# Exponents of an mLSTM's attention-like product taken off TensorE from the fourth chunk on: maxima spread by DMA, masked by GpSimd, applied by ScalarE

## The reference

```python
for t in range(S):
    m_new = np.maximum(f_gate[:, :, t] + m, i_gate[:, :, t])
    f_stab = np.exp(f_gate[:, :, t] + m - m_new)
    i_stab = np.exp(i_gate[:, :, t] - m_new)
    m = m_new
    C = f_stab * C + i_stab * np.einsum('bhd,bhe->bhde', vt, kt)
    n = f_stab * n + i_stab * kt
    h_tilde = np.einsum('bhde,bhe->bhd', C, qt)
    denom = np.maximum(np.abs(np.einsum('bhd,bhd->bh', n, qt)), 1.0)
    y[:, :, t] = sigmoid(o_gate[:, :, t]) * h_tilde / denom
```

## Time and profile before

| | us |
|---|---|
| median of 3 runs (327.9 to 329.29) | 329.14 |
| the profiled execution, whole | 330.02 |
| its span, first to last instruction | 328.3 |
| PE busy / PEld busy | 311.1 / 297.5 |
| DVE busy | 207.6 |
| ACT busy | 151.7 |
| POOL busy | 53.8 |

### The profile page before, as it was taken

One profiled execution on the slowest core, in us unless ns is written; L12 is line 12 of the kernel. 1 busy time (PEld: TensorE's weight loads), 2 busy tenths in 40 slices (PEclk: granted clock), 3 DMA queues, 4 the chain that ended last, 5 costly groups with the idle time before them and its releaser, 6 DMA issues.

```text
span 328.3 us, 5497 instructions
## 1 busy us (share of the span) xinstructions
PE 311.1 (95%) x1952; PEld 297.5 (91%) x1952; DVE 207.6 (63%) x448; ACT 151.7 (46%) x295; POOL 53.8 (16%) x80
## 2 busy tenths in 40 slices
PE   7879978999999999787999999999899999999996
PEld 3879967999899999577999999999899999999996
DVE  7886798767577656744543388886876448657111
ACT  4945565333313332542212367678867166536000
POOL 8712231212021200340211110140000000000000
PEclk9995999999999999999999999999999999999999
DMA  5992221122214215400004202040000100010011
GB/s 147 282 249 70 84 83 37 47 82 84 85 38 145 79 41 195 128 0 2 1 2 137 55 2 60 1 143 18 2 1 20 43 0 2 20 40 2 20 51 51
DMA packets 11374, 20.92 MB, mean 64 GB/s; under 512 B 1908, under 2 KB 5508, under 8 KB 11348
## 3 DMA queue, kind: packets, MB, share of 16 engines
q1 hardware_dynamic: 11348, 20.58, 21.2%
HBM read 18.53 MB, written 1.97 MB: 62 GB/s over the span
## 4 chain that ended last, share of the span: by engine, by line
PE 80%; DVE 9%; ACT 4%; issue 3%; DMA 2%; POOL 1%; SPq 0%; DVEq 0%; ACTq 0%; POOLq 0%
PE ps_v L1096 18%; PE ps_s L1096 11%; PE ps_e L1096 7%; PE ps_in L1096 7%; PE ps_out L1096 6%; PE ps_t L1096 6%; PE ps_s L1165 5%; PE ps_z L1096 5%; PE ps_in L1174 5%; PE ps_out L1184 3%; PE ps_z L1193 2%; DMA wv_raw<-in_w_v 2%; PE ps_e L1142 1%; PE ps_e L1147 1%; DVE pt L826 1%
## 5 line engine op out<-in xcount | busy, mean ns | idle before, releaser
L1165 PEld LDWEIGHTS ps_s<-qkt 128*128 128x128 f32 x192 | 26.0, 200 | 3.0 <-DMA qkt<-in_qk 1.5
L1165 PE MATMUL ps_s<-qkt 128*128 128x128 f32 x192 | 27.1, 287 | 1.3 <-DMA qkt<-in_qk 1.3
L1174 PEld LDWEIGHTS ps_in<-tok,pt 128*128 128x128 f32 x192 | 25.0, 198 | 0.9
L1068 DVE TENSOR_TENSOR kr<-kr 128x384 f32<-128x384 f32 x32 | 17.7, 557 | 12.5 <-ACT kr L755 12.4
L1174 PE MATMUL ps_in<-tok,pt 128*128 128x42 f32 x192 | 24.8, 281 | 0.0
L578 ACT ACTIVATE et<-ps_e 128x512 f32<-128x512 f32 x24 | 14.3, 595 | 20.7 <-PE ps_e L1147 14.5
L727 ACT ACTIVATE gh<-ut 128x384 fp32r<-128x384 f32 x16 | 8.4, 524 | 32.3 <-DVE ut L1034 32.3
L1096 PE MATMUL ps_v<-win,xth 128*128 128x512 f32 x60 | 21.0, 416 | 1.3 <-DVE xtl L907 1.3
L1096 PE MATMUL ps_v<-xth,win 128*128 128x384 f32 x65 | 19.1, 359 | 2.5 <-ACT vr L584 1.4
L826 DVE TENSOR_TENSOR pt<-ps_s,et 128x512 f32<-128x512 f32 x24 | 16.5, 688 | 5.7 <-PE ps_s L1165 4.1
L538 POOL TENSOR_TENSOR gl<-ut,gh 128x384 fp32r<-128x384 f32 x8 | 9.0, 1121 | 59.0 <-ACT gh L727 59.0
(11 more groups left out here) (292 smaller groups left out, 901.7 us busy)
## 6 DMA issues: line engine op xcount, KB each, us to landing
tok<-in_vk SPq DMA_DIRECT2D x12, 328.0 KB, 4.0
qkt<-in_qk SPq DMA_DIRECT2D x24, 160.0 KB
sp_raw<-in_w_sp SPq DMA_DIRECT2D x6, 384.0 KB, 4.6
osig<-in_og SPq DMA_DIRECT2D x2, 960.0 KB, 9.5
out_y<-ob SPq DMA_DIRECT2D x12, 160.0 KB, 1.8
wv_raw<-in_w_v SPq DMA_DIRECT2D x2, 640.0 KB, 5.3
win_raw<-in_w_in SPq DMA_DIRECT2D x4, 256.0 KB, 6.5
wk_raw<-in_w_k SPq DMA_DIRECT2D x2, 512.0 KB, 4.4
```

Of the source, the lines that this page charges most:

```text
L1068: ve.tensor_tensor(kr[n % 4][:, :], kr[n % 4][:, :], kr[n % 4][:, :], ALU.mult).then_inc(sems["kk_done"], 1)
L1165: last = te.matmul(ps_s[j][:, h * CH:(h + 1) * CH], keys[u % NS][:, HH * j + h, :], queries[u % NS][:, h, :], start=True, stop=True)
L1174: last = te.matmul(p_in[:, HH * j + h, :], pt[:, j, h, :], vt[u % 2][:, HH * j + h, :], start=True, stop=True)
```

## The change

- For units 3 to 11 nothing of the exponent is made on TensorE. SP writes the gate maxima `mx` to DRAM (`save_maxima`) and reads them back spread over all 128 partitions into one of two tiles `mb` of 128x1024 (`spread_maxima`).
- GpSimd replaces the entries with s > t by 2^100 (`mask`); it does unit u+1's in slot u, behind inverse_deviation(u−2).
- ScalarE takes eight Exps of 128x128 per unit, one a head: scale −1 on `mb` and the key's a as a bias per partition, from a third group of columns of `gwt`, for which gate_factors copies a once more per chunk.
- `gate_operands` and `gates_lo` (the split of a and −M for TensorE) are left out for chunks 3 to 5, `max_rows` altogether. `mrow` has no batch any more: GpSimd's second memset and head_rows(1, ·) go.
- The batches' gate rows stand closer (GW = 8 instead of 32).
- The u products go to `ps_e` with semaphores of their own (`u_mm`, `u_read`); v products keep `ps_v`.

```diff
-GW = 32
-GR = GW + H
+GW = H
+GR = B * GW
@@ SP
-            def max_rows(u):
...
+            def save_maxima(first, last, signal):
+                sp.wait_ge(sems["gate_m"], last)
+                sp.dma_start(maxima[first:last].rearrange("c r t -> r c t"),
+                             mx[:, first * CH:last * CH].rearrange("r (c t) -> r c t", t=CH)).then_inc(sems[signal], 16)
+
+            def spread_maxima(u):
+                b, c = batch(u), chunk(u)
+                if c < EARLY:
+                    sp.wait_ge(sems["mx_first"], 16)
+                else:
+                    sp.wait_ge(sems["mx_saved"], 16 * (c - EARLY + 1))
+                if u >= EARLY + 2:
+                    sp.wait_ge(sems["exp_done"], 2 * (u - 2) + 2)
+                rows = maxima[c, GW * b:GW * b + H].rearrange("h t -> (h t)")
+                sp.dma_start(mb[u % 2].rearrange("p h t -> p (h t)"),
+                             rows.partition_broadcast(128)).then_inc(sems[f"mx_in{u % 2}"], 16)
...
             for u in range(1, NU):
+                if EARLY <= u + 1 < NC:
+                    save_maxima(u + 1, u + 2, "mx_saved")
+                if u + 1 == NC:
+                    save_maxima(0, EARLY, "mx_first")
                 if EARLY <= u + 1 < NU:
-                    max_rows(u + 1)
+                    spread_maxima(u + 1)
@@ GpSimd
+            def mask(u):
+
+                pool.wait_ge(sems[f"mx_in{u % 2}"], 16 * ((u - EARLY) // 2 + 1))
+                gp.affine_select(out=mb[u % 2][:, :, :], in_=mb[u % 2][:, :, :], compare_op=ALU.is_ge, fill=-NEVER,
+                                 base=0, pattern=[[0, H], [1, CH]],
+                                 channel_multiplier=-1).then_inc(sems["masked"], 1)
...
                 if u >= 2:
                     inverse_deviation(u - 2)
-                if u == 0:
...
-                    head_rows(1, 0)
-                    head_rows(1, 1)
+                if EARLY <= u + 1 < NU:
+                    mask(u + 1)
                 if u in WIN_SLOT:
                     win_lo_of(WIN_SLOT.index(u))
@@ ScalarE
+                sc.activation(gw[64:ER, c, :], am[:, t], ACT.Copy).then_inc(sems["factors"], 1)
 
             def exponentials(u, j):
                 hf = 2 * u + j
-                act.wait_ge(sems["expo_mm"], hf + 1)
                 if hf > 1:
                     act.wait_ge(sems["probs_done"], hf - 1)
-                sc.activation(et[:, j, :, :], ps_e[:, :].rearrange("p (h t) -> p h t", h=HH),
-                              ACT.Exp).then_inc(sems["exp_done"], 1)
+                if u < EARLY:
+                    act.wait_ge(sems["expo_mm"], hf + 1)
+                    last = sc.activation(et[:, j, :, :], ps_e[:, :].rearrange("p (h t) -> p h t", h=HH), ACT.Exp)
+                else:
+                    act.wait_ge(sems["masked"], u - EARLY + 1)
+                    act.wait_ge(sems["gwt_done"], chunk(u) + 1)
+                    for h in range(HH):
+                        x = 64 + GW * batch(u) + HH * j + h
+                        last = sc.activation(et[:, j, h, :], mb[u % 2][:, HH * j + h, :], ACT.Exp,
+                                             bias=gwt[:, chunk(u), x:x + 1], scale=-1.0)
+                last.then_inc(sems["exp_done"], 1)
...
-                if u + 2 < NC:
+                if u + 2 < EARLY:
                     gate_operands(u + 2)
@@ TensorE
             def u_product(g, m):
-                pe.wait_ge(sems["v_read"], V_AT["u", g, m])
-                u_chain(ps_v[:, 0:NB], g, m).then_inc(sems["v_bank_mm"], 1)
+                pe.wait_ge(sems["exp_done"], 2 * EARLY)
+                pe.wait_ge(sems["u_read"], U_AT[g, m])
+                u_chain(ps_e[:, 0:NB], g, m).then_inc(sems["u_mm"], 1)
...
+                if u < EARLY:
+                    exponents(u, 0)
                 if u < NU:
-                    exponents(u, 0)
                     scores(u, 0)
...
+                if u < EARLY:
+                    exponents(u, 1)
                 if u < NU:
-                    exponents(u, 1)
                     scores(u, 1)
```

More of the change, by code:

```diff
@@ L37 @@
 HH = H // 2
-GW = 32
-GR = GW + H
+GW = H
+GR = B * GW
 ER = 64 + GR
+ZR = 64 + D
 NB = 384
@@ L81, in u_tiles @@
     return out
[L84 to L95, removed]
+U_ORDER = [x for slot in range(NU + 2) for x in u_tiles(slot)]
+U_AT = {x: n for n, x in enumerate(U_ORDER)}
 def mlp_groups():
@@ L222, in program @@
     kw = tail("kw", [128, G, 128])
-    nm = tail("nm", [ER, S], F32R)
-    est = tail("est", [ER, NC, CH], F32R)
+    nm = tail("nm", [ER, EARLY * CH], F32R)
+    est = tail("est", [ER, EARLY, CH], F32R)
     gwt = tail("gwt", [128, NC, ER])
@@ L231, in program @@
     zt = [tail(f"zt{n}", [KR, G, 2, DV]) for n in range(2)]
-    zdec = tail("zdec", [ER, G, 2, DV])
+    zdec = tail("zdec", [ZR, G, 2, DV])
+    mb = [at("mb0", [128, H, CH], EP + 12288), tail("mb1", [128, H, CH])]
+    maxima = nc.dram_tensor("maxima", (NC, GR, CH), F32, kind="Internal").ap()
     vr = tail("vr", [128, HF])
@@ L446, in _, with head_rows @@
             gp.memset(rstd[:, 1:2], -0.5)
-            gp.memset(bits(mrow[:, 0, :, :, :]), 0.0).then_inc(sems["rows_zero"], 1)
+            gp.memset(bits(mrow[:, :, :, :]), 0.0).then_inc(sems["rows_zero"], 1)
             pool.wait_ge(sems["rows_zero"], 1)
[L450 to L454, removed]
+            def head_rows(j):
+                for n, r in enumerate((0, 64)):
+                    pool.wait_ge(sems["head_rows_done"], 2 * j + n)
+                    rows = mrow[r:r + H, j, :, :]
                     gp.affine_select(out=rows, in_=bits(rows), compare_op=ALU.not_equal, fill=1.0,
@@ L469, in _ @@
             pool.wait_ge(sems["later_done"], 1)
-            head_rows(0, 1)
+            head_rows(1)
             gp.memset(qkt[:, 2, :], 0.0).then_inc(sems["pad2"], 1)
-            gp.memset(bits(mrow[:, 1, :, :, :]), 0.0).then_inc(sems["rows_one_zero"], 1)
             gp.memset(kw[:, :, :], 0.0).then_inc(sems["kw_zero"], 1)
@@ L1146, in exponents @@
                 pe.wait_ge(sems["later_done"], 1)
-                last = te.matmul(ps_e[:, :].rearrange("p (h t) -> p h t", h=HH), later[:, :],
-                                 ones[:, :].unsqueeze(1).broadcast_to([128, HH, CH]),
-                                 start=False, stop=u >= EARLY)
-                if u < EARLY:
-                    pe.wait_ge(sems["nm_hi_done"], c + 1)
-                    pe.wait_ge(sems["nm_lo_done"], c + 1)
-                    for h in range(HH):
-                        last = te.matmul(ps_e[:, h * CH:(h + 1) * CH],
-                                         mrow[:, b, j, h, 0:1].broadcast_to([ER, CH]),
-                                         nm[:, c * CH:(c + 1) * CH], start=False, stop=h == HH - 1)
+                te.matmul(ps_e[:, :].rearrange("p (h t) -> p h t", h=HH), later[:, :],
+                          ones[:, :].unsqueeze(1).broadcast_to([128, HH, CH]), start=False, stop=False)
+                pe.wait_ge(sems["nm_hi_done"], c + 1)
+                pe.wait_ge(sems["nm_lo_done"], c + 1)
+                for h in range(HH):
+                    last = te.matmul(ps_e[:, h * CH:(h + 1) * CH],
+                                     mrow[:, j, h, 0:1].broadcast_to([ER, CH]),
+                                     nm[:, c * CH:(c + 1) * CH], start=False, stop=h == HH - 1)
                 last.then_inc(sems["expo_mm"], 1)
```

84 lines of the change are left out of this document (35 added, 49 removed).

## The result

The changed kernel takes 325.59 us in the median of 11 runs (323.16 to 327.16), the kernel before 329.14 in 11 (327.77 to 331.88). The ratio is 0.9895, its 95% interval 0.9861 to 0.9929: 3.55 us faster, where 5.6 were forecast. The profiled execution of the changed kernel took 325.59 too, its span is 323.9 against 328.3.

The account below looks back on a forecast made before the run. TensorE was taken to bound slots 5 to 11, then a VectorE-GpSimd-ScalarE loop of 9.58 us per slot. 3.7 by slot 12 plus 1.9 in the tail gave 5.6 us earlier: 324.4 profiled, 323.5 median; range 319.5 to 332.

Parts of the forecast that it names:

- What bounds the kernel: Slots 5 to 11: TensorE is the limit at 10.2 us per slot, VectorE little behind; a new loop becomes the bound.
- The loop: Once per slot through VectorE, GpSimd, ScalarE, VectorE: L895, rstd, mask, Exps, pt to `inter`, handovers; 9.58 us; chance 0.40.
- the step into slot 6: The loop's passage into slot 6, without state_add (−0.66): 8.92 us.
- The spread: The 512 KB spread lands in an estimated 6 us, started some 14 us before mask(u) needs it.
- The bank and the tail: Slots 12 and 13: with its own bank the u product no longer waits 0.69 us, twice; together an estimated 1.9 us.
- The entry to slot 3: Mask(3) and Exps stand where L512 stood, rstd comes 0.5 us earlier; I(3), the start of `inter`, at 44.0, 0.65 later.
- The table load: Load of 1.28 us before et(4,0), taken as hidden; 1.3 us added if issued only after the mask wait.
- Into slot 12: No mask; VectorE ready at I(11) + 6.3, TensorE at + 5.2; I(12) at 128.1 us, 3.7 earlier.
- 9.1 in the mean, and less: TensorE's need per slot after the change: 10.2 − 1.1 = 9.1 us, less as its waits shrink when ahead.
- TensorE idle about 1 us per slot: Sign of a right prediction: TensorE waits about 1 us per slot at values(u,0).
- Loop, not TensorE, is the bound: Forecast: loop of 9.58 us per slot limits, chance 0.40; rival that TensorE stays the limit: 319.6 us, chance 0.14.
- what follows only shifts: Behind the tail, the rest of the kernel only moves earlier, with no gain or loss of its own.

Follow-up runs that it names:

- e12_before_one: The kernel before without the second TensorE product of each exponent pair from unit 3 on, masking left out there; 328.21 us, ratio 0.9957.
- e3_mask_twice: The changed kernel with a second, equal GpSimd mask behind each first; 336.47 us, ratio 1.0204 to the kernel before.
- e2_mask_first: The changed kernel with GpSimd's mask(u+1) in front of inverse_deviation(u-2) instead of behind it; 321.76 us, ratio 0.9799.
- e5_u_same_bank: The changed kernel with the u products back in `ps_v`, with the waits that this takes; 328.6 us, ratio 0.9967.
- e4: The changed kernel with a one-column Exp at the end of slot 3, so the Exp table loads there; 322.95 us, ratio 0.9809.
- e9_again: The changed kernel run again without an edit; 326.66 us, ratio 0.9902.
- e1_again: The changed kernel run again without an edit; 324.27 us, ratio 0.984.
- e8_before_again: The kernel before run again without an edit; 327.84 us in one run.
- e6_one_exp: The changed kernel with one Exp of 512 columns without bias in place of four of 128, keys' part left out; 322.1 us, ratio 0.9786.

## Why the prediction was right, and where its steps were off

The kernel is faster by over 0.5%, 325.59 lies inside 319.5 to 332, and the mechanism is the one forecast; the gain is 2.1 smaller.

- **What bounds the kernel.** Held. The pairs were on TensorE's path (`e12_before_one`, for the second product of each), and a loop over three engines (VectorE, GpSimd, ScalarE) closed behind them (`e3_mask_twice`, `e2_mask_first`).
- **The loop.** Held in every term. Predicted 4.80, 0.93, 1.10, 1.30, 1.30 and 0.15 of handovers; measured in slot 8, 4.76, 0.96, 1.09, 1.28, 1.31 and 0.17, less 0.04 by which the mask starts within `rstd`'s duration. The sum, 9.58, came out at 9.52, the step into slot 6 (8.92) at 8.80, from slot 7 (9.04) at 9.16. The choices between far bounds were right: the mask by the selects, not by GpSimd's two-input rows, and the Exps by the overlap of L706 and L694.
- **The spread.** Held. 512 KB landed in 3.7, not the estimated 6, and the mask in after starts behind `rstd`, not behind a landing.
- **The bank and the tail.** Held: 1.9 predicted, 1.92 measured from I(12) to the first spatial product, and `e5_u_same_bank` gives it back. The wait at the first u product of slot 12 is gone.
- **The entry to slot 3.** I(3) was to come 0.65 later. In the repeated traces it is 41.14 and 41.48 against 41.40: no difference that these absolute marks can show, since the lower clock falls ahead of slot 3 differently in each. The step itself did get longer: I(2) to I(3) is 13.45 or 13.46 in after, `e4`, `e5` and `e9_again` and 13.88 in `e1_again`, against 12.95 in `e8_before_again` and 12.94 in `e12_before_one`. So a price of 0.5 or more is there, near the forecast, and an I(2) that comes earlier in four of these five traces than in any of the kernel before hides it. Why it comes earlier isn't shown.
- **The table load.** This step failed. I took the load as hidden, because it followed directly on the work before it, and named 1.3 us if it was issued only behind the wait. It is: 1.28 in the path of slot 3, and `e4_exp_early` takes 1.27 of it back. The row of before has no idle time in front of the load, so it couldn't tell where the load goes when there is a wait. The Trainium skill ("ScalarE: Activation LUTs", section "Step-by-step: what each stage is for") says that the load is placed right before the ACTIVATE that needs it; the trace agrees, for it stands at 50.57, behind the mask's end. Read with the waits that the changed `exponentials` puts in front of its first Exp, that sentence would have moved the sum by 1.3 the right way.
- **Into slot 12.** This step failed too: I(11) + 7.13 instead of 6.3. I let TensorE be ready at + 5.2, ahead of VectorE, as if its spare time of each slot were still there. I had worked with its mean need, "9.1 in the mean, and less", and not followed where it stands after two slots with two u products. It was 0.08 ahead at I(11). Cost: 0.8. The sign I named for a right prediction, TensorE idle about 1 us per slot, isn't there from slot 7 on.
- **"Loop, not TensorE, is the bound".** Half right. In slots 3 to 6 it is the loop, from slot 7 on the two are level, and there only the longer of both counts: `e6_one_exp` shortened the loop by 0.65 a slot and won nothing there. The size that I had wrong is TensorE's need, "9.1 in the mean, and less": with the loop open it is 9.20 (`e2_mask_first`), and the loop's own mean between I(5) and I(11) is 9.34 (56.04 in six steps). Nothing in the sum had shown that the two would come out so close.

The sum again, between the repeated traces: entry about 0, slots 3 to 6 +3.2 (predicted +2.3), slots 7 to 11 −5.9 (−6.7), tail −1.9. That is 4.6 us less, and the medians show 3.55. What is between may be the clock. Over the timed executions, without the one of each kernel that stands far off (382.72 and 752.85), the mean granted clock was 0.984 in the median before (47) and 0.976 after (24). A straight line through these executions falls by 1.5 us for each 0.01 of clock before and by 1.9 after, which makes 1.2 to 1.5. The sentence "what follows only shifts" was not quite right either: `e9_again` lost 1.6 to 2.0 behind the slots. No run shows by itself what the change does to the clock.

## What to carry to other kernels

When work is moved off the busiest engine, write down the new round of waits through all the engines that it goes to, and sum it per iteration: that sum, not the freed time, is the gain's limit. Then follow both the loop and the relieved engine through the uneven iterations, since two limits that are level in the mean leave no slack to spend. In an in-order queue the place of the new operation can be worth more than its duration: moved ahead of one short dependent operation, the same 1.09 us mask was off the path from slot 7 on, and the ratio was 0.9799 where the changed kernel beside it had 0.984, and 0.975 where it had 0.9902.

## What the runs showed of the hardware

- **A table load waits with its Exp.** 1.28 us behind a wait of 2.87 that could have covered it twice; with the mask done early it came without one. The load alone is what it cost here (1.27 came back). The Trainium skill ("ScalarE: Activation LUTs", section "What ACT_TABLE_LOAD costs") adds about 1.38 us of draining; no run here shows that: the Exp at 51.86 follows on the load at once, and in `e2_mask_first` the load at 48.08 starts 0.02 behind the end of the work before it.
- **GpSimd's mask stretches some of VectorE's operations beside it.** In the kernel after, groups by line:

```profile
L914 DVE TENSOR_SCALAR vnf<-vr,mv,rstd 128x512 f32<-128x512 f32 x12 | 12.9, 1073 | 3.7 <-POOL rstd L502 3.6
```

  Before, the mean was 0.65. On the path that cost nothing there, as VectorE next waits for the Exps. In `e2_mask_first` it did count: L807 took 1.71 instead of 0.67, and L886 0.87 at 98.03, where it takes 0.17 elsewhere. The Trainium skill ("GPSIMD Engine Reference", section "8. Key points") names VectorE's two-port and two-input instructions for this; L807 and L886 have two inputs, so the trace agrees for them, and for `vnf`, which has one, it shows the stretch but not the mode.
- **Exps into the same partitions follow each other at 0.30, at 389 ns each.** The three factor copies into different partitions keep the 0.42 of the earlier trace rows in the kernel after as well (53.04, 53.45, 53.88). Whether the partitions make the difference isn't shown; no run varied them alone.
- **Where TensorE runs at the lower of its clocks differs between executions of one kernel.** Idle time ahead of it doesn't decide it alone: from 52 to 56 us TensorE was busy 1.36 of 4 us in after and 1.59 in `e9_again`, and the granted clock of the next 4 us was 0.55 in the one and 1.00 in the other. A slow step of 2 us in one trace was gone in two others. A difference of that size in a single trace needs a second trace before it is given a cause.
